# A three-stage attention and feed-forward kernel: queries and probabilities turned by VectorE and moved by DMA in place of TensorE transposes

## The reference, cut to what matters

```python
k_p = k.reshape(B, H, Sp, 8, D).mean(axis=3)          # Sp = 72
v_p = v.reshape(B, H, Sp, 8, D).mean(axis=3)
scores = scale * np.matmul(q, k_p.transpose(0, 1, 3, 2))
attn = np.exp(scores - max);  attn = attn / (sum + 1e-09)
x = np.matmul(attn, v_p)                              # then (B*S, H*D) = 4608 x 512
h = x @ w_in;  g = where(h >= 1, h, where(h <= -1, 0, (h + 1)**2 / 4));  y = g @ w_out
h = y @ w_in2; g = h * sigmoid(h);                    return g @ w_out2
```

## Time and profile before

| | |
|---|---|
| median of three runs | 1781.04 us |
| the profiled execution | 1778.62 us, span 1776.8 us |
| TensorE (PE) busy | 1732.1 us, 97% |
| DVE, POOL, ACT busy | 715.8, 542.5, 475.6 us |
| DMA queue of SP | 92.49 MB, 17.9% of 16 engines |
| chain that ended last | PE 92%, DVE 5% |

### The profile page before, as it was taken

One profiled execution on the slowest core, in us unless ns is written; L12 is line 12 of the kernel. 1 busy time (PEld: TensorE's weight loads), 2 busy tenths in 40 slices (PEclk: granted clock), 3 DMA queues, 4 the chain that ended last, 5 costly groups with the idle time before them and its releaser, 6 DMA issues.

```text
span 1776.8 us, 21342 instructions
## 1 busy us (share of the span) xinstructions
PE 1732.1 (97%) x8000; PEld 1401.7 (79%) x8000; DVE 715.8 (40%) x987; ACT 475.6 (27%) x784; POOL 542.5 (31%) x410
## 2 busy tenths in 40 slices
PE   6699999999999999999999999999999999999998
PEld 4477778777778787878888788888888888888887
DVE  3577555555555555645357422121211112121211
ACT  2243222222222222222123422232222222222222
POOL 4633443425234342432222222222222222222222
PEclk9799999999999999999999999999999999999999
DMA  6333222221213122121023301010101010101000
GB/s 152 84 106 112 63 74 66 62 69 48 79 55 81 53 76 69 47 80 51 0 66 95 120 5 48 0 47 0 47 0 47 0 47 0 47 12 36 16 8 24
DMA packets 87799, 92.96 MB, mean 52 GB/s; under 512 B 47988, under 2 KB 47988, under 8 KB 87764
## 3 DMA queue, kind: packets, MB, share of 16 engines
q1 hardware_dynamic: 87764, 92.49, 17.9%
HBM read 65.21 MB, written 27.26 MB: 52 GB/s over the span
## 4 chain that ended last, share of the span: by engine, by line
PE 92%; DVE 5%; ACT 1%; issue 1%; DMA 1%; SPq 0%; DVEq 0%; ACTq 0%
PE ps_y L543 14%; PE ps_h L543 14%; PE ps_y L544 14%; PE ps_y L545 14%; PE ps_h L545 14%; PE ps_h L544 14%; PE ps_a L498 2%; PE ps_a L517 2%; PE ps_a L478 1%; PE ps_a L453 1%; DVE wout_lo L858 1%; DVE g_tmp L916 1%; DVE g_tmp L919 0%; DVE g_tmp L914 0%; PE ps_a L491 0%
## 5 line engine op out<-in xcount | busy, mean ns | idle before, releaser
L991 POOL TENSOR_TENSOR g_lo<-g_tmp,g_hi 128x512 fp32r<-128x512 f32 x288 | 375.5, 1304 | 1187.3 <-ACT g_hi L761 1187.3
L543 PE MATMUL ps_h<-x_hi,win_hi 128*128 128x512 f32 x1144 | 454.4, 397 | 13.0 <-DVE x_lo L904 11.7
L545 PE MATMUL ps_h<-x_hi,win_lo 128*128 128x512 f32 x1144 | 447.5, 391 | 0.0
L544 PE MATMUL ps_h<-x_lo,win_hi 128*128 128x512 f32 x1144 | 447.4, 391 | 0.0
L923 DVE TENSOR_TENSOR g_tmp<-g_tmp,ps_h 128x512 f32<-128x512 f32 x144 | 99.0, 688 | 585.8 <-ACT g_tmp L757 585.8
L761 ACT ACTIVATE g_hi<-g_tmp 128x512 fp32r<-128x512 f32 x288 | 182.0, 632 | 505.1 <-DVE g_tmp L919 389.3
L543 PEld LDWEIGHTS ps_h<-x_hi,win_hi 128*128 128x128 f32 x1144 | 215.7, 189 | 67.3 <-issue 22.9
L545 PEld LDWEIGHTS ps_h<-x_hi,win_lo 128*128 128x128 f32 x1144 | 216.0, 189 | 45.8
L544 PEld LDWEIGHTS ps_h<-x_lo,win_hi 128*128 128x128 f32 x1144 | 216.1, 189 | 42.6
L543 PE MATMUL ps_y<-g_hi,wout_hi 128*128 128x512 f32 x576 | 231.4, 402 | 8.3 <-DVE g_tmp L919 7.2
L544 PE MATMUL ps_y<-g_lo,wout_hi 128*128 128x512 f32 x576 | 226.2, 393 | 0.0
(11 more groups left out here) (86 smaller groups left out, 1308.2 us busy)
## 6 DMA issues: line engine op xcount, KB each, us to landing
kv_raw<-in_k_dram SPq DMA_DIRECT2D x16, 576.0 KB
y_dram<-y_sb SPq DMA_DIRECT2D x36, 256.0 KB, 2.1
x_raw<-y_dram SPq DMA_DIRECT2D x18, 512.0 KB, 4.3
out_dram<-y_sb SPq DMA_DIRECT2D x36, 256.0 KB, 2.1
q_pair<-in_q_dram SPq DMA_DIRECT2D x68, 128.0 KB, 2.4
kv_raw<-in_v_dram SPq DMA_DIRECT2D x15, 576.0 KB
x_raw<-x_dram SPq DMA_DIRECT2D x16, 512.0 KB, 3.8
w_raw<-in_moe_w_in_dram SPq DMA_DIRECT2D x28, 256.0 KB, 4.1
```

The source lines that it names most:

```text
L543: mm(dst, w_h, a_h, start=first, stop=False)
L544: mm(dst, w_h, a_l, start=False, stop=False)
L545: return mm(dst, w_l, a_h, start=False, stop=last)
L991: nc.gpsimd.tensor_tensor(g_lo[:, s % G_BUFS, :], g_tmp[:, s % T_BUFS, :], g_hi[:, s % G_BUFS, :].bitcast(F32), ALU.subtract).then_inc(g_l ...
```

## The change

Queries of later batches are loaded as 32 x 32 squares (four DMAs a pair with rows of 32 numbers, eight for the tail) and one DVE transpose of squares puts them in `qT`. The probabilities are padded to 96 columns; one DVE transpose puts the squares into `prob_sq`, which lies in the upper half of x_raw, and 12 DMAs (6 for the tail) from SBUF to SBUF bring them to the partitions of their keys, in `pT`. TensorE's Q and T pieces and ACT's copies of them are gone, except for batch 0. S of unit u is in slot 5u instead of 5u + 3, Q in 5u + 3, K in 3 instead of 6, V stays in 5u + 7. The ring of weights has 5 places at first instead of 7, and SP's order changes.

```diff
-RING = 7
+RING = 5
...
 UNITS = 5
-PIECES = {0: [("Q", 0)], 6: [("T", 0), ("K", 0)], 7: [("V", 0), ("Q", 1)], 3: [("S", 0)]}
-for _u in range(1, UNITS):
-    PIECES.setdefault(3 + 5 * _u, []).append(("S", _u))
-    PIECES.setdefault(6 + 5 * _u, []).append(("T", _u))
-    PIECES.setdefault(7 + 5 * _u, []).append(("V", _u))
-    if _u + 1 < UNITS:
-        PIECES.setdefault(7 + 5 * _u, []).append(("Q", _u + 1))
+PIECES = {3: [("Q", 0), ("K", 0)]}
+for _u in range(UNITS):
+    PIECES.setdefault(5 * _u, []).append(("S", _u))
+    PIECES.setdefault(5 * _u + 7, []).append(("V", _u))
+    if _u > 0:
+        PIECES.setdefault(5 * _u + 3, []).append(("Q", _u))
+PAD = 96
+SPAN = 32
...
-FIRST_SLOTS = [[3], [4], [], [5, 6], [7], [8, 9]]
+FIRST_SLOTS = [[0], [1], [], [2, 3], [4], [5, 6, 7, 8]]
...
         if s < AHEAD + 2:
             return [], FIRST_SLOTS[s]
...
         kT = sb("kT", [P, PAIRS, 2, keys])
         qT = sb("qT", [P, BLOCK])
-        prob = sb("prob", [P, 2, 4, keys])
...
-                   .rearrange("p (r c k) -> p r c k", r=2, k=keys)]
-        row_max = sb("row_max", [P, 2, 4])
-        row_sum = sb("row_sum", [P, 2, 4])
...
+        row_den = sb("row_den", [P, 2 * TILES])
+        row_inv = sb("row_inv", [P, 2 * TILES])
+        pT = sb("pT", [keys, 4, 2 * P])
+        pT_early = pT.rearrange("k i c -> k (i c)").rearrange("k (r t) -> k r t", r=2)
         ident = sb("ident", [P, P])
+        prob_sq = x_raw[:, 2:4, :].rearrange("p c n -> p (c n)")[:, 0:2 * TILES * PAD]
...
             def load_q(at, c):
                 for r in range(2):
-                    src = q[at, 2 * c + r, 0:BLOCK].rearrange("(t p) d -> p t d", p=P)
-                    sp.dma_start(q_pair[:, c % 2, :, r, :], src).then_inc(q_landed[c % 2], 16)
+                    for j in range(dim // SPAN):
+                        src = q[at, 2 * c + r, 0:BLOCK, j * SPAN:(j + 1) * SPAN]
+                        rows = slice((2 * r + j) * SPAN, (2 * r + j + 1) * SPAN)
+                        dst = q_pair[rows, c % 2, :].rearrange("p (i d) -> p i d", d=SPAN)
+                        sp.dma_start(dst, src.rearrange("(i p) d -> p i d", p=SPAN)
+                                     ).then_inc(q_landed[c % 2], 16)
             def load_q_tail(at):
-                src = q[at, :, BLOCK:seq].rearrange("h p d -> p h d")
-                sp.dma_start(q_tail[:], src).then_inc(q_tail_landed, 16)
+                for r in range(2):
+                    for j in range(dim // SPAN):
+                        rows = slice((2 * r + j) * SPAN, (2 * r + j + 1) * SPAN)
+                        for i in range(TAIL // SPAN):
+                            tokens = slice(BLOCK + i * SPAN, BLOCK + (i + 1) * SPAN)
+                            src = q[at, r:heads:2, tokens, j * SPAN:(j + 1) * SPAN]
+                            dst = q_tail[rows, :].rearrange("p (c i d) -> p c i d", i=2, d=SPAN)
+                            sp.dma_start(dst[:, :, i, :], src.rearrange("c p d -> p c d")
+                                         ).then_inc(q_tail_landed, 16)
+            def move_probs(b, u):
+                sp.wait_ge(prob_turned, 5 * b + (u + 1))
+                for i in range(4 if u > 0 else 2):
+                    for j in range(PAD // SPAN):
+                        n = min(SPAN, keys - j * SPAN)
+                        src = prob_sq[i * SPAN:i * SPAN + n, j * 2 * P:(j + 1) * 2 * P]
+                        sp.dma_start(pT[j * SPAN:j * SPAN + n, i, :], src).then_inc(pT_landed, 16)
...
             def attention_dmas(b, after, weights=lambda i, j: None):
                 n = b + 1
-                sp.wait_ge(qT_made, unit(b, 0))
                 load_q_tail(n)
-                weights(14, 18)
-                store_tail(b)
-                sp.wait_ge(qT_made, unit(b, 1))
+                if isinstance(b, int):
+                    sp.wait_ge(o_made, PAIRS)
+                move_probs(b, 0)
+                sp.wait_ge(q_turned, 5 * b + 2)
                 load_q(n, 2)
+                weights(15, 16)
                 sp.wait_ge(kv_added, 12 * b + 9)
                 load_kv(v, n, 1)
-                weights(18, 22)
+                store_tail(b)
+                move_probs(b, 1)
+                weights(16, 20)
+                sp.wait_ge(q_turned, 5 * b + 3)
+                load_q(n, 3)
                 store_pair(b, n, 0)
-                sp.wait_ge(qT_made, unit(b, 2))
-                load_q(n, 3)
+                move_probs(b, 2)
                 sp.wait_ge(kv_added, 12 * b + 12)
                 load_kv(k, after, 0)
-                weights(22, 26)
+                weights(20, 26)
+                sp.wait_ge(q_turned, 5 * b + 4)
+                load_q(after, 0)
                 store_pair(b, n, 1)
-                sp.wait_ge(qT_made, unit(b, 3))
-                load_q(after, 0)
+                move_probs(b, 3)
+                weights(26, 30)
                 sp.wait_ge(kv_added, 12 * b + 15)
                 load_kv(k, after, 1)
-                weights(26, W_PIECES)
+                sp.wait_ge(q_turned, 5 * b + 5)
+                load_q(after, 1)
+                weights(30, W_PIECES)
                 load_x(b + 1, x_dram, b + 1, 0, 80 * b + 48)
                 store_pair(b, n, 2)
-                sp.wait_ge(qT_made, unit(b, 4))
-                load_q(after, 1)
+                move_probs(b, 4)
                 sp.wait_ge(kv_added, 12 * b + 18)
                 load_kv(v, after, 0)
                 store_pair(b, n, 3)
...
-            first_weights(3, 7)
+            first_weights(3, 5)
...
             load_q_tail(0)
-            first_weights(7, 9)
+            first_weights(5, 9)
             sp.wait_ge(qT_made, 3)
             load_q(1, 0)
             first_weights(9, 12)
@@ -394,7 +440,7 @@
             load_kv(k, 1, 1)
             sp.wait_ge(qT_made, 4)
             load_q(1, 1)
-            first_weights(12, 14)
+            first_weights(12, 15)
             sp.wait_ge(kv_added, 6)
             load_kv(v, 1, 0)
@@ -403,6 +449,7 @@
             with sp.Fori(1, batches - 1) as b:
                 attention_dmas(b, (b + 2) % batches)
                 store_y(b, b, 0)
+            move_probs(batches - 1, 0)
             store_tail(batches - 1)
...
             def turn_keys(b, u):
                 pe.wait_ge(kv_added, 12 * b + 6)
+                pe.wait_ge(scores_taken, unit(b, 0))
...
-            def turn_queries(b, u):
-                if u == 0:
-                    pe.wait_ge(q_tail_landed, 16 * b + 16)
...
             def scores(b, u):
-                pe.wait_ge(qT_copied, unit(b, u))
+                pe.wait_ge(q_turned, 5 * b + (u + 1))
                 if u > 0:
-                    pe.wait_ge(o_copied, 5 * b + u)
+                    pe.wait_ge(o_copied, 5 * b + (u - 1))
+                    if u == 1:
+                        pe.wait_ge(kT_copied, 2 * b + (2 * PAIRS + 2))
                     pair_scores(ps_a, u - 1)
                     return
+                pe.wait_ge(o_copied, 5 * b)
...
+                              start=True, stop=True)
+                last.then_inc(o_made, 1)
+            def values(b, u):
+                pe.wait_ge(pT_landed, 864 * b + (192 * u + 96))
+                if u + 1 < UNITS and not (isinstance(b, int) and b == batches - 1):
+                    pe.wait_ge(scores_taken, unit(b, u + 1))
                 if u > 0:
-                    turn_pair_probs(prob)
+                    pe.wait_ge(kv_added, 12 * b + (9 + 3 * ((u - 1) // 2)))
+                    pair_values(u - 1, pT.rearrange("k i c -> k (i c)")
+                                .rearrange("k (a r c) -> k r a c", r=2, c=SPAN))
                     return
                 pe.sem_inc(tail_ready, 1)
-                for r in range(2):
-                    for c in range(PAIRS):
-                        at = (r * PAIRS + c) * TAIL
-                        last = nc.tensor.transpose(ps_a[0:keys, 0, at:at + TAIL], prob[0:TAIL, c // 2, 2 * (c % 2) + r, :],
-                                                   ident[0:TAIL, 0:TAIL])
-                last.then_inc(pT_made, 1)
...
             def first_block():
-                attention_slot(0, 3, UNITS)
+                attention_slot(0, 0, UNITS)
                 hidden(0, AHEAD, 0)
                 output(0, 0, 0, 0)
                 output(0, 1, 0, 0)
-                attention_slot(0, 6, UNITS)
                 hidden(0, AHEAD + 1, 0)
+                attention_slot(0, 3, UNITS)
+                output(0, 2, 0, 0)
+                attention_slot(0, 5, UNITS)
+                output(0, 3, 0, 0)
                 attention_slot(0, 7, UNITS)
-                output(0, 2, 0, 0)
-                attention_slot(0, 8, UNITS)
-                output(0, 3, 0, 0)
...
+            def turn_probs(b, u):
+                rows = P if u > 0 else TAIL
+                dve.wait_ge(prob_made, unit(b, u))
+                if u > 0:
+                    dve.wait_ge(pT_landed, 864 * b + (192 * u - 96))
```

(72 more changed lines are left out.)

80 lines of the change are left out of this document (42 added, 38 removed).

## The result

The changed kernel takes 1783.49 us, the median of 12 runs (1782.56 to 1786.83), against 1779.59 (1777.42 to 1782.67) for the kernel before in as many runs beside it: ratio 1.0022, interval 1.0014 to 1.0030. It is slower by 3.9 us (0.2%, clear of the noise), where 1766 was forecast. The two traces differ by 6.0 us of span (1782.8 against 1776.8), and the mean granted clock fell from 0.990 to 0.977.

The account below looks back on a forecast made before the run. TensorE, busy 97% of the span, was taken to bound the kernel. Blocks 1 to 6 -31.8, the last block -1.0 and block 0 +18 sum to -14.8 us: from 1781.04 to 1766, range 1748 to 1786.

Parts of the forecast that it names:

- The saving of TensorE in blocks 1 to 6: Query and probability pieces taken from TensorE save 6.5 us a block.
- The stall at unit 1's scores: Blocks 1 to 6: TensorE waits there for ACT's key copies behind gate 1, 1.2 us a block.
- The period: Length of a repeated block, 1 to 6: 105.0 less 6.5 plus 1.2, so 99.7 us.
- DVE's transposes: On DVE, 0.95 us for 768 columns and 0.69 for 512, bounded by half and twice that.
- rival 2: Long DVE transposes stall TensorE 2.2 us at unit 1's scores and lower the clock: 1785 us, chance 0.13.
- rival 3: Moves run serially, each paid in full, every block at least 128 us: near 1942 us, chance 0.02.
- rival 4: No stall at unit 1 because keys come earlier, block 0 as forecast: 1759 us, chance 0.13.
- rival 1: Block 0 doesn't hang on the moves and costs 3 us at most: 1751 us, chance 0.17.
- block 0, +18 forecast: Weights behind moves in SP's queue lengthen block 0 by 15.6 us, plus 2.4 for the clock.
- the bound of +28: Block 0's upper bound, if each link is a microsecond longer; a worse block 0 had chance 0.10.
- 12 issues take 5.9 us: A pair's moves on SP's queue, 0.49 us each as for query loads; with landing about 8.2.
- I add 2.4: Block 0: 2.4 us added because long stalls halve the clock, most of that lying inside later waits.

Follow-up runs that it names:

- experiment 3: The changed kernel with block 0's weights issued ahead of the moves and, in later blocks, keys copied and unit 1's queries turned ahead of gate 1: 1746.88 us.
- experiments 7 and 8: The kernel before with only the queries loaded as squares and turned by DVE: 1772.74 us; the kernel before with only the ring of five: 1779.54 us.
- experiment 5: The changed kernel with four more small DMAs among each pair's moves in blocks 1 to 6 only: 1794.26 us.
- experiment 1: The changed kernel with block 0's weights issued ahead of the moves in SP's queue, the DMAs themselves the same: 1753.9 us.

## Why the prediction was wrong

**What held.** The saving of TensorE in blocks 1 to 6: 6.5 forecast, 6.46 in experiment 3. The stall at unit 1's scores: 1.2 forecast, 1.0 in its row, 1.23 when taken away. The period: 99.7 forecast, 99.77 measured. DVE's transposes: 0.95 and 0.69 forecast, 0.98 and 0.70 measured, in these rows of a steady block:

```profile
338.50 0.98 DVE L905 STREAM_TRANSPOSE x_raw<-prob 128x768 f32<-128x768 f32 x1
341.42 0.70 DVE L913 STREAM_TRANSPOSE qT<-q_pair 128x512 f32<-128x512 f32 x1
```

So rival 2's mechanism (slow transposes) is refuted, and so are rival 3 (a period of 99.77, not 128), rival 4 (the stall is there) and rival 1 (block 0 costs 34).

**What failed: block 0, +18 forecast, +33.9 measured**, beyond the bound of +28. The places were right: the 5.2 at the tail's values (5 forecast), waits before hidden chunk 8, at unit 3's scores and at a later weight. Their sizes were not. The step that failed is the one that priced a round of block 0's loop: "12 issues take 5.9 us", from query loads at 0.49; a weight landing "2.8 later"; weight 19 split 1 us behind the taking of scores 2; and "I add 2.4" for the clock. The moves go from partitions to partitions of SBUF and take 0.63 with the gap, 7.6 for twelve; the weight behind them lands after 3.3, 5.8 and 3.7; the splits behind scores 2 take 4.0; the clock costs some 6.5. In the forecast's own times the error grows from round to round:

```
                                forecast   measured
kv_added                          110.3      108.2
moves of unit 1 issued            116.9      117.1
scores 2 taken                    125        126.0
weight 19 split                   126        130.05
hidden chunk 8                    126.3      130.1
moves of unit 2 issued            138        143.3
the weight behind them landed     141        149.7
scores 3                          146        154.4
wait for weight 27                3          6.6
block 1 starts                    196        212.0
```

In round 1 the moves were issued on time by luck: POOL was done 2.1 us early, and that hid their longer issue. Chunk 8 is 3.8 late for what follows, mainly the splits of weights 18 and 19, which stand on ACT and DVE behind the exponential and the taking of scores 2:

```profile
127.31 2.74 DVE L868 TENSOR_TENSOR win_lo<-w_raw,win_hi 128x512 fp32r<-128x512 f32 x2 [1.27 <-ACT win_hi L717]
```

Round 2 adds 4.6 (8.4 late at scores 3): 1.7 more of issue, 0.5 for the load of keys, 3.0 more of landing, less 0.6 elsewhere. Round 3 adds 3.6 at weight 27: again 1.7 of issue, 0.9 of landing, and the rest for the weight issued ahead of it and small steps. That is 12.0 us, and the idle time agrees: the forecast was 22.1 us of new idle time (15.6 and the saving of 6.5), measured are 34.0, 11.9 more. The other 4 are the clock. TensorE is busy 104.98 us as before with 55 matmul records fewer, at 0.82 instead of 0.91: if the saving of 6.5 is in block 0 as in the others, the clock cost some 6.5 (an estimate, by difference), not 2.4. After the wait of 14.14 the eight score matmuls take 2.29; at 110.65 and 171.92, with no wait before them, 1.14. 11.9 and 4.1 are the 15.9 that were missing. The upper bound of +28 was too low for the same reasons: it allowed 10 us over all links, a microsecond each, and named no more for the clock.

The case that came, a block 0 worse than +28, was given a chance of 0.10. That 1783.5 lies inside the range and close to rival 2's 1785, and that block 0 is above the +33 which rival 2 named as its sign, is luck: its mechanism, slow transposes, is not there.

**The smaller misses.** Block 1 was forecast like the others; it takes 102.63, for the wait of 2.27 at the tail's keys and a fallen clock behind it (0.98 over the block). The end was forecast 1.0 shorter and is 0.6 longer. From block 7 on TensorE waits three times (1.22, 1.33 and 1.18, together 3.73), before twice (1.15 and 0.91, together 2.06): 1.67 more, the size of the miss. The new one is at block 8's third hidden chunk. Its gate stands on DVE behind the copy of `y_sb`, which waited 4.44 us for a store to land, 2.92 before:

```profile
906.83 0.69 DVE L968 COPY y_sb<-ps_y 128x512 f32<-128x512 f32 x1 [4.44 <-DMA y_dram<-y_sb]
...
909.62 0.50 PE L567 MATMUL ps_h<-x_hi,win_hi 128*128 128x512 f32 x1 [1.22 <-DVE g_tmp L953]
```

All runs with the moves have this wait (0.50 to 1.22), and the three kernels without them (before, experiments 7 and 8) don't. Why the stores of `y_sb` come free later is not shown. The cover of the moves, "3 us", was 1.4 at most; it cost nothing here, and experiment 5 shows how near it was.

The order that makes this so stood in the diff, and the prediction named it. What it lacked was a check of the sum's lever: an issue price taken from another kind of DMA, multiplied by 36 on a loop of dependence, and the engines' own order behind each landing.

The Trainium skill ("DMA: Bandwidth & Descriptors", Issuing engines are not separate DMA queues) says that the time a sequencer takes to start a DMA is usually small beside the DMA itself. Here a single move takes 0.51 to 0.66 us of SP's queue; when a move lands the profile doesn't show, so the ratio is not tested. What counts here is the sum: 7.6 us to issue twelve moves, and experiment 1 took 29.4 us off block 0 with nothing changed but what is issued first.

## What to carry to other kernels

In this kernel a DMA cost its place in the issuing queue before it cost bandwidth. When many small transfers join an in-order queue, list what stands behind them, and issue ahead of them whatever feeds the engine that releases them. Price an issue by a row of the same kind of transfer, and if the issues lie on a loop (moves, weights, split, gate, next moves), multiply by the number of rounds before setting bounds (here 3.8 us of time for each microsecond of a pair's issue). Follow each landing through the engines that work on it: a split that stands behind another unit's work came 4 us later, not 1. A steady-state gain of 5 us a block is real and can be given back whole in the one block where weights stream; look at the two stages apart.

## What the runs showed that was not expected

Issue times on SP's queue differ by transfer: 0.33 to 0.43 us for most weights of 128 partitions of 2 KB (one, at 181.83, took 3.31), 0.51 to 0.66 for an SBUF-to-SBUF move (0.59 each when all have 32 partitions, so fewer partitions don't make it cheaper). The eight of w_in between 110 and 182 us (ns, least, median, most):

```profile
L288 SPq DMA_DIRECT2D w_raw<-in_moe_w_in_dram x8: 327/430/435, 117.1 to 174.4; - x8
```

DVE's transposes of 4-byte elements take 0.70 us for 512 columns, as the gate's instructions of that width do (0.69), and 0.98 for 768.

In the windows inside the two longest waits of the changed kernel's block 0, 120 to 126 and 148 to 154, TensorE is idle and the granted clock is 0.51 and 0.50, the lower of its two levels (1.2 of 2.4 GHz); from 173 to 179 it still reads 0.93.
